# Recurrent attention and two expert layers on one core: the second batch's heads of a pair change places, and the start of the program is re-ordered

## The reference

```python
for t in range(S):                      # S = 768, per batch and head, D = 48
    y[t] = r[t] @ (state + (u * k[t]) outer v[t])
    state = w[t][:, None] * state + k[t] outer v[t]
...
x = y as 3072 rows of 384
h = x @ w_in                            # 384 -> 2048
x = (h * clip(h + 3, 0, 6) / 6) @ w_out # 2048 -> 384
xn = x / sqrt(mean(x * x) + 1e-6) * rms_g
x = (silu(xn @ w_gate) * (xn @ w_val)) @ w_out2   # 384 -> 1536 -> 384
```

## Time and profile before

| | us |
|---|---|
| median of 3 runs | 956.05 |
| lowest, highest | 953.65, 956.09 |
| the profiled execution's own time | 953.81 |
| its span | 952.1 |

### The profile page before, as it was taken

The page is one execution under the profiler, slowest core; times in us unless marked ns, Lnnn a source line. Parts: engine busy times, 40 slices in busy tenths (PEclk is TensorE's granted clock), DMA queues, the critical chain, the costliest instruction groups (busy, mean ns, idle before and its releaser), DMA issues.

```text
span 952.1 us, 17493 instructions
## 1 busy us (share of the span) xinstructions
PE 934.7 (98%) x7060; PEld 782.7 (82%) x7060; DVE 538.8 (57%) x781; ACT 358.1 (38%) x756; POOL 304.8 (32%) x246
## 2 busy tenths in 40 slices
PE   7899999999999999999999999999999999999998
PEld 7789988888888888888788888888888888888887
DVE  8897986667666676313784463463373373363332
ACT  4446544444444445435464123223223222313212
POOL 5687654455445454422561011011001101102000
PEclk9999999999999999999999999999999999999999
DMA  9855433223323222004222000010000001000000
GB/s 238 239 173 143 117 94 95 59 60 104 89 68 92 62 72 80 17 9 143 84 82 67 1 34 34 1 34 33 1 33 34 1 1 66 1 1 34 1 1 33
DMA packets 32927, 60.19 MB, mean 63 GB/s; under 512 B 6096, under 2 KB 19920, under 8 KB 32848
## 3 DMA queue, kind: packets, MB, share of 16 engines
q1 hardware_dynamic: 27392, 51.67, 18.9%
q10 hardware_dynamic: 5456, 7.41, 2.6%
HBM read 47.46 MB, written 9.44 MB: 60 GB/s over the span
## 4 chain that ended last, share of the span: by engine, by line
PE 88%; DVE 4%; ACT 3%; issue 2%; POOL 2%; DMA 1%; SPq 0%; ACTq 0%; DVEq 0%; POOLq 0%
PE acc L1051 32%; PE bank L1035 11%; PE bank L1037 11%; PE bank L1036 11%; PE pair L1036 5%; PE pair L1035 5%; PE pair L1037 5%; PE pair L1157 2%; DVE cum L682 1%; PE pair L1104 1%; PE acc L1247 1%; PE pair L1133 1%; PE bank L1125 1%; ACT att L501 1%; DVE ki L706 1%
## 5 line engine op out<-in xcount | busy, mean ns | idle before, releaser
L1051 PE MATMUL acc<-gs,w_dn 128*128 128x512 f32 (+1 forms) x1512 | 357.1, 382 | 0.7 <-POOL gs L928 0.7
L1051 PEld LDWEIGHTS acc<-gs,w_dn 128*128 128x128 f32 x1512 | 273.0, 188 | 55.0 <-POOL gs L928 0.9
L928 POOL TENSOR_TENSOR gs<-act_g,gs 128x512 fp32r<-128x512 f32 (+1 forms) x96 | 122.2, 1273 | 208.2 <-ACT gs L535 208.0
L1035 PE MATMUL bank<-xs,w_up 128*128 128x512 f32 (+1 forms) x480 | 180.1, 375 | 5.1 <-DMA xs<-y 1.4
L1037 PE MATMUL bank<-xs,w_up 128*128 128x512 f32 (+1 forms) x480 | 176.5, 368 | 0.0
L1036 PE MATMUL bank<-xs,w_up 128*128 128x512 f32 (+1 forms) x480 | 176.5, 368 | 0.0
L769 DVE SCALAR_TENSOR_TENSOR act_g<-act_u,bank 128x512 f32<-128x512 f32 (+1 forms) x112 | 68.0, 607 | 131.9 <-ACT act_u L527 131.0
L839 DVE TENSOR_TENSOR act_u<-act_u,bank 128x512 f32<-128x512 f32 x72 | 49.5, 687 | 149.2 <-ACT act_u L595 149.2
L527 ACT ACTIVATE act_u<-bank,half 128x512 f32<-128x512 f32 (+1 forms) x112 | 70.0, 625 | 137.9 <-PE bank L1037 137.8
L1035 PEld LDWEIGHTS bank<-xs,w_up 128*128 128x128 f32 x480 | 90.4, 188 | 23.2 <-DVE act_g L769 2.9
L599 ACT ACTIVATE gs<-act_g 128x512 fp32r<-128x512 f32 x72 | 45.5, 632 | 158.8 <-DVE act_g L845 158.8
(11 more groups left out here) (119 smaller groups left out, 1152.4 us busy)
## 6 DMA issues: line engine op xcount, KB each, us to landing
rkt<-in_rkT SPq DMA_DIRECT2D x48, 192.0 KB, 3.7
rkn<-in_rkN SPq DMA_DIRECT2D x22, 384.0 KB, 4.2
val<-in_valN SPq DMA_DIRECT2D x22, 256.0 KB, 3.0
dec<-in_decT SPq DMA_DIRECT2D x48, 97.5 KB, 2.7
x<-x_dram SPq DMA_DIRECT2D x6, 768.0 KB, 4.3
x_dram<-xo SPq DMA_DIRECT2D x5, 768.0 KB, 4.1
out<-xo SPq DMA_DIRECT2D x5, 768.0 KB, 3.2
raw_dn<-in_w_out SPq DMA_DIRECT2D x14, 192.0 KB, 4.5
```

Source lines behind the costliest of these rows:

```text
L928: pool.tensor_tensor(gs[:, f % GRING, 1, tok], act_g[:, f % 2, tok], gs[:, f % GRING, 0, tok].bitcast(F32), ALU.subtract).then_inc(s_glo, 1)
L1035: pe.matmul(dst, w_hi, x_hi, start=first, stop=False)
L1051: last = pe.matmul(ps_o[m][:, tok], w[:, wp, m * P:(m + 1) * P], gs[:, f % GRING, xp, tok], start=f == 0 and a == 0, stop=f == nf - 1 and ...
```

## The change

Three things.

1. In the second batch (b = 1) the two heads of a pair change places in everything that lies transposed or is summed per head (dec, rkt, and therefore cum, ki, rd, state, scores, att, bonus). Index i is now the place, and the head at it is i ^ b. The host lays out the inputs so; val and the outputs keep their order. `across` reads at the partitions of place i and writes at those of head i ^ b, so it uses all four quarters. It is no longer split: all 16 matmuls stand behind sums(g). bonuses(g) needs a u_h for each batch and so has 8 matmuls of 64 columns instead of 4 of 128, and u_b is loaded in two halves.
2. The start: SP issues only the four dec transfers and rms_s ahead of its wait; the four rkt transfers come from ACT's queue, ahead of u_h; val(0) and val(1) are issued behind u_h and ACT's first activation; ACT's wait for rkt(0) ahead of the weights is gone. `diag` and `mask` are made by ACT in four copies of 64 x 64 instead of by DVE in three instructions.
3. busy(24) becomes busy(18), busy(4) becomes busy(3).

```diff
-        NCONST = 4
+        NCONST = 5
...
                 for j in (1, 0):
-                    if g < 2 and j == 0:
-                        sp.wait_ge(zeroed[g], 1)
                     sp.dma_start(rkt[HI2 * j:HI2 * j + D, slot(g), :, :, :, :], rkT[g // SETS, g % SETS, j]).then_inc(ldR[slot(g)], 16)
...
             for g in range(2):
                 load_dec(g)
-                load_rk(g)
             sp.dma_start(rms_s[:, :], rms_g).then_inc(ldG, 16)
             landed(sp, ldR, 1, 2)
-            sp.dma_start(u_b[:, :], u.partition_broadcast(P)).then_inc(ldU, 16)
+            for b in range(PB):
+                sp.dma_start(u_b[T * b:T * (b + 1), :], u[b].partition_broadcast(T)).then_inc(ldU, 16)
...
             for g in range(2):
-                act.dma_start(val[:, g, :, :], valN[0, g]).then_inc(ldV[g], 16)
-            act.dma_start(u_h[0:DP, :, :], u_heads).then_inc(ldH, 16)
+                for j in (1, 0):
+                    if j == 0:
+                        act.wait_ge(zeroed[g], 1)
+                    act.dma_start(rkt[HI2 * j:HI2 * j + D, g, :, :, :, :], rkT[0, g, j]).then_inc(ldR[g], 16)
+            act.dma_start(u_h[0:DP, :, :, :], u_heads).then_inc(ldH, 16)
             act.wait_ge(s_half, 1)
             act.activation(y3[:, 0, 0:1], half[:, :], ACT.Copy)
-            landed(act, ldR, 0, 2)
+            for g in range(2):
+                act.dma_start(val[:, g, :, :], valN[0, g]).then_inc(ldV[g], 16)
+            for made, to, of in ((s_ident, diag, ident), (s_upper, mask, upper)):
+                act.wait_ge(made, 1)
+                for b in range(PB):
+                    rows = slice(T * b, T * (b + 1))
+                    act.activation(to[rows, :], of[rows, T * b:T * (b + 1)], ACT.Copy).then_inc(const, 1)
...
-            dve.wait_ge(s_ident, 1)
-            dve.tensor_tensor(diag[:, :], ident[:, 0:T], ident[:, T:P], ALU.add).then_inc(const, 1)
-            dve.wait_ge(s_upper, 1)
-            for b in range(PB):
-                rows = slice(T * b, T * (b + 1))
-                dve.tensor_copy(mask[rows, :], upper[rows, T * b:T * (b + 1)]).then_inc(const, 1)
...
-                                         val[T * b:T * (b + 1), q, 2 * p + j, 0:D], start=True, stop=True, skip_group_check=True)
+                                         val[T * b:T * (b + 1), q, 2 * p + (i ^ b), 0:D], start=True, stop=True, skip_group_check=True)
...
-                    last = pe.matmul(bonus_bank(g)[:, 2 * p:2 * p + 2], rk_t[g][0:DP, p, :], u_h[0:DP, p, :], start=True, stop=True)
+                    for b in range(PB):
+                        last = pe.matmul(bonus_bank(g)[T * b:T * (b + 1), 2 * p:2 * p + 2], rk_t[g][0:DP, p, T * b:T * (b + 1)],
+                                         u_h[0:DP, p, b, :], start=True, stop=True, skip_group_check=True)
...
-            def across(g, tiles):
-
+            def across(g):
+
+                pe.wait_ge(p_in, g + 1 - PLACED)
+                state_taken(pe, g - SETS)
                 for p in range(PAIRS):
-                    for j, b in tiles:
-                        rows = slice(HI2 * j, HI2 * j + D)
-                        last = pe.matmul(y_of(g)[rows, b, p * T:(p + 1) * T], state[rows, g % SETS, p, b, :],
+                    for i, b in TILES:
+                        rows = slice(HI2 * i, HI2 * i + D)
+                        heads = slice(HI2 * (i ^ b), HI2 * (i ^ b) + D)
+                        last = pe.matmul(y_of(g)[heads, b, p * T:(p + 1) * T], state[rows, g % SETS, p, b, :],
                                          rd[rows, slot(g), p, b, :], start=False, stop=True, skip_group_check=True)
-                return last
+                last.then_inc(p_y, 1)
...
                 last.then_inc(p_in, 1)
-                state_taken(pe, g - SETS)
-                across(g, TILES[0:2])
...
                 if g >= PLACED:
-                    pe.wait_ge(p_in, g + 1 - PLACED)
-                    across(g, TILES[2:4]).then_inc(p_y, 1)
+                    across(g)
...
-            busy(24)
+            busy(18)
...
-            busy(4)
+            busy(3)
```

More of the change, by code:

```diff
@@ L118, in build @@
         val3 = sa("val3", [P, PLACED, 2, KT, HI2])
-        u_h = sa("u_h", [P, PAIRS, 2])
+        u_h = sa("u_h", [P, PAIRS, PB, 2])
         last = sa("last", [P, LASTS, PAIRS * PB])
@@ L1005, in _ @@
                 split_up(f)
-            pool.wait_ge(ldU, 16)
+            pool.wait_ge(ldU, 16 * PB)
             rku_mul(2)
@@ L1101, in scores @@
                 for p in range(PAIRS):
-                    for j, b in TILES:
-                        rows = slice(HI2 * j, HI2 * j + D)
-                        last = pe.matmul(scores_of(g)[T * b:T * (b + 1), j, p * T:(p + 1) * T], ki[rows, q, p, b, :],
+                    for i, b in TILES:
+                        rows = slice(HI2 * i, HI2 * i + D)
+                        last = pe.matmul(scores_of(g)[T * b:T * (b + 1), i, p * T:(p + 1) * T], ki[rows, q, p, b, :],
                                          rd[rows, q, p, b, :], start=True, stop=True, skip_group_check=True)
@@ L1122, in sums @@
                 for p in range(PAIRS):
-                    for b, j in TILES:
-                        rows = slice(HI2 * j, min(HI2 * (j + 1), DP))
+                    for b, i in TILES:
+                        rows = slice(HI2 * i, min(HI2 * (i + 1), DP))
                         last = pe.matmul(sum_bank(g, b)[rows, p * D:(p + 1) * D], kiT[T * b:T * (b + 1), p, rows],
-                                         val[T * b:T * (b + 1), q, 2 * p + j, 0:D], start=True, stop=True, skip_group_check=True)
+                                         val[T * b:T * (b + 1), q, 2 * p + (i ^ b), 0:D], start=True, stop=True, skip_group_check=True)
                 last.then_inc(p_st, 1)
@@ L1133, in inside @@
                     last = pe.matmul(y_of(g)[HI2 * j:HI2 * (j + 1), b, p * T:(p + 1) * T], val[T * b:T * (b + 1), q, 2 * p + j, :],
-                                     att[T * b:T * (b + 1), q, j, p, :], start=p == 0, stop=False, skip_group_check=True)
+                                     att[T * b:T * (b + 1), q, j ^ b, p, :], start=p == 0, stop=False, skip_group_check=True)
                 return last
@@ L1140, in inside3 @@
                     last = pe.matmul(y_of(g)[HI2 * j:HI2 * (j + 1), b, k * T:(k + 1) * T], val3[T * b:T * (b + 1), g, j, k, :],
-                                     att[T * b:T * (b + 1), g, j, PAIRS - 1, :], start=False, stop=True, skip_group_check=True)
+                                     att[T * b:T * (b + 1), g, j ^ b, PAIRS - 1, :], start=False, stop=True, skip_group_check=True)
                 return last
@@ L1280, in chunks_transposed, with swapped, heads_of_u, chunks_swapped @@
     def chunks_transposed(x):
-        x = x.reshape(SETS, PB, PAIRS, 2, NT, T, D).transpose(4, 0, 3, 6, 2, 1, 5)
+        x = x.reshape(SETS, PB, PAIRS, 2, NT, T, D)
+        x = np.stack([x[:, 0], x[:, 1, :, ::-1]], axis=1).transpose(4, 0, 3, 6, 2, 1, 5)
         return np.ascontiguousarray(x)
+    def swapped(heads):
+        heads = heads.reshape(PAIRS, 2, D)
+        return np.stack([heads, heads[:, ::-1]])
+    def heads_of_u(u):
+        u = np.einsum("bpid,ij->idpbj", swapped(u), np.eye(2, dtype=np.float32))
+        u = np.pad(u, ((0, 0), (0, HI2 - D), (0, 0), (0, 0), (0, 0)))
+        return np.ascontiguousarray(u.reshape(P, PAIRS, PB, 2)[:DP])
+    def chunks_swapped(x):
+        x = x.reshape(SETS, PB, PAIRS, 2, NT, T, D)
+        x = np.stack([x[:, 0], x[:, 1, :, ::-1]], axis=1).transpose(4, 0, 1, 5, 2, 3, 6)
+        return np.ascontiguousarray(x).reshape(NT, SETS, C, DM)
     def chunks_natural(x):
@@ L1308 @@
         "valN": np.pad(chunks_natural(inputs["v"]), ((0, 0),) * 5 + ((0, HI2 - D),)).reshape(NT, SETS, C, H * HI2),
-        "rkN": np.stack([chunks_natural(inputs[n]).reshape(NT, SETS, C, DM) for n in "rk"], axis=3).reshape(NT, SETS, C, 2 * DM),
-        "u_heads": np.pad(np.einsum("pjd,ji->jdpi", inputs["u"].reshape(PAIRS, 2, D), np.eye(2, dtype=np.float32)),
-                          ((0, 0), (0, HI2 - D), (0, 0), (0, 0))).reshape(P, PAIRS, 2)[:DP],
-        "u": np.ascontiguousarray(inputs["u"]).reshape(DM),
+        "rkN": np.stack([chunks_swapped(inputs[n]) for n in "rk"], axis=3).reshape(NT, SETS, C, 2 * DM),
+        "u_heads": heads_of_u(inputs["u"]),
+        "u": np.ascontiguousarray(swapped(inputs["u"])).reshape(PB, DM),
         "w_in": into_slices(rows_of_x1(inputs["moe_w_in"])), "w_out": out_slices(inputs["moe_w_out"]),
```

3 lines of the change are left out of this document (2 added, 1 removed).

## The result

| | before | after |
|---|---|---|
| median (five executions each) | 954.69 | 948.20 |
| lowest, highest | 953.23, 956.09 | 946.26, 950.51 |
| profiled execution: own time, span | 953.81, 952.1 | 946.26, 944.5 |

The ratio is 0.9922, 95% interval 0.9904 to 0.9939: faster by 0.6 to 1.0%. The medians lie 6.5 us apart, the two profiled executions 7.55. The median of 956.05 from which the prediction counts was that of three executions; five have 954.69. Two executions took more than three times as long as the others, one of before (3300.02) and one of e12 (3310.72); they are counted in the medians and left out of the ratios.

The account below looks back on a forecast made before the run. PE was taken to bound from 130 to 420 us, and DVE work to hold it at the start; 6.2 + 0.4 + 0.9 + 2.0 = 9.5 off the median 956.05 gave 946.5 us, range 941 to 951.

Parts of the forecast that it names:

- across on four quarters: In each meet on PE, sums, across and drain take 1.00 us instead of 1.44, saving 0.44 (0.32 to 0.50).
- the part on the start: Earlier dec landing and an undisturbed second scan leave 2.0 us gained at 125 us (0.5 to 2.5).
- the sum of 6.2 + 0.4: Gain in PE's full stretch: 6.2 us from groups 8 to 21, 0.4 from groups 22 and 23.
- Groups 22 and 23: Meets without sums: across waits for inside's semaphore, yet each saves 0.2 us, both 0.4 (0 to 0.6).
- no overlap: Rival: in across, row halves sharing a bank go one after the other, nothing gained per meet; 954.0 us, 12%.
- one at a time: Rival: bank sharing makes each across matmul wait for the one before; slower, 968 us, 4%.
- landed at 4.4: At the start, dec(0) lands at 4.4 us, so the first scan on DVE gains 1.3 (0 to 1.4).
- The step on the second scan: Group 1's scan on DVE no longer stands behind POOL's multiply: 1.24 us instead of 2.30, 1.06 gained.
- PE's first up: PE's first up, at 22.56 us before, comes at most 2.3 earlier, near 20.3.
- the early meets: Groups 2 to 7 count only where the wait chain goes through PE, twice: 0.9 us (0 to 2.6).
- The start gives nothing: Rival: dec still lands at 5.6 us and rkt(1) late, so the start gains nothing; 948.5 us, 15%.

Follow-up runs that it names:

- e12: The kernel before with the new start alone, plus busy(8) and 15 unread filler matmuls in PE's start gaps; median 956.06 us, ratio 0.9996 to before.
- e8: The kernel after with another order of place and batch in across, so neighbours write the same bank from both row halves; 948.98 us.
- e5: The kernel after with ACT's first rkt transfer held until both dec(0) transfers have landed; median 949.65 us, ratio 0.994 to before.
- e1: The kernel after with the start and both busy counts as before, so the new layout and across only; median 947.85 us, ratio 0.9922 to before.
- e2: The kernel before with the new start alone, including busy(18) and busy(3); median 959.10 us, ratio 1.0032 to before.
- e4: The kernel before with all 16 across matmuls moved behind sums, still on two quarters; median 957.92 us, ratio 1.0033 to before.
- e6: The kernel after with diag and mask made by DVE again; 949.22 us.

## Why the prediction was right

The forecast was 946.5 in 941 to 951; 948.2 came out, faster. The gain is less well met than the time: 9.5 were forecast from a median of 956.05, and the medians of five lie 6.5 apart. Two thirds of the forecast (6.6 of 9.5) were right for their reason, across on four quarters; the part on the start was not, and that the time lies in the range all the same is owed to the range, which takes in a start that gives nothing. By its steps:

- **Across on four quarters.** Right in mechanism and size: 0.43 a meet against 0.44. Between pass 2 and pass 6 the sum of 6.2 + 0.4 came out as 5.82, 0.8 less. The period from one meet to the next, 226.47 - 207.04 = 19.43 before and 221.36 - 202.33 = 19.03 after, shrank by 0.40, so some 0.03 of each meet's 0.43 went back into the steps behind it. That is the part mis-sized: 14 x 0.40 = 5.6, and twice 0.13 for the groups below.
- **Groups 22 and 23.** From inside to the down, group 22 took 0.47 + 0.99 = 1.46 and takes 394.00 - 392.67 = 1.33: 0.13 gained for 0.2 forecast, with a gap of 0.26; group 23 gains 0.13 too (1.51 before, 1.38 after).
- **The banks.** The rivals "no overlap" (954.0) and "one at a time" (968) fell with the meet of 2.00 and with e8.
- **The start.** The step "landed at 4.4" failed: rkt's transfers moved beside dec, and it landed for a scan at 5.47 (e5: 3.84 with them held back). Of the 1.3 only 0.2 came. The step on the second scan was right (1.23 against 1.24 forecast, 1.07 gained), but I had overlooked ki(0) between them: from the end of the reciprocals to the second scan it is 11.38 - 10.13 = 1.25 instead of 11.05 - 10.34 = 0.71, since POOL's multiply of rkt(1), now from 9.65 to 10.91, has begun ahead of ki(0), which stands behind it and takes 1.22. (In before ki(0) began first, at 10.44 against 10.48, and took 0.69.) 0.20 + 1.07 - 0.54 = 0.73, so ki(1) began at 16.13, not 14.5. PE's first up came at 20.92, not 20.3. At pass 2 3.13 were gained against 2.9 forecast for start and early meets, but that they agree is luck: 1.05 of it goes with the clock of the two executions, the early meets gave 0.44 for 0.9, and the first up's 1.64, for 2.0, has the clock in it as well.
- **What that was worth.** In the one profiled execution the 2.0 seemed nearly right; in the medians it isn't there. e1, without the new start, has 947.85, and e2, with the new start alone, is 3 us slower than before. "The start gives nothing", 948.5, which had 15%, describes the median better than the forecast's sum does. What I had not named is PE's own instruction supply, and the clock beside it: the chain of waits of before shows neither, since in that execution the packet came at 16.76 and in time.
- **The sum.** In the profiled pair it closes: 3.13 + 5.82 - 1.40 = 7.55. The forecast of 9.5 was 1.95 too high there: 0.8 by groups 8 to 23, 1.4 by the reload of x, less 0.2 that stretches with unlike clocks gave more. It closes by number, not by cause.

Open are why the instruction packet comes late in some executions and whether the new start has to do with it, and why e2 is behind before, and e12 level with it, where the full change is not behind e1.

## What to carry to other kernels

When small matmuls use quarters of the array, look at which index sets the row half and which the column half: a host layout in which two indices cross (i ^ b) makes two quarters into four, and the starts of records, not their lengths, price it beforehand. A gain at a saturated start must be tested by itself and in several executions, since one profile can show a stretch at its best. And a stop of PE between two matmuls of one line, with no engine named, can be tested by counting instructions up to it in two kernels: the same count, and an instruction packet that starts shortly ahead of the end of the stop, mean that the instructions were late. And before a gain between two profiles is put down to a change, compare their granted clocks: one fall of 3.4 us was worth 1.6 us.

## What the runs showed of the hardware

- PE stood for 0.58 to 4.45 us in front of the same instruction by count in eight of fourteen profiled executions, and went on 2.5 to 2.9 us behind the start of the first 16 KB instruction packet (15.2 to 21.3 us).
- A fall of the granted clock to 0.50 for 3.4 us cost 1.6 us where PE was full (516.7 instead of 515.1 in e4 and e6), and 1.0 to 1.1 from 31.5 us (e6 and e8 against after).
- Two row halves wrote one bank on different partitions at full pace: 30 records and the drain in 0.56.
- The 16 narrower records of bonuses(0) start from 10.0 to 10.4, the 8 wide ones of before from 11.2 to 11.9: weight loads of 0.138 instead of 0.192 us.
- DVE's scan or ki and a POOL product of two operands in SBUF did not run side by side; the one that began later stood until the other ended. Scan behind POOL: 2.30 (before) and 2.21 (e5) instead of 1.23; ki(0) behind POOL: 1.22 (after) instead of 0.69; POOL behind DVE: 1.77 (before) and 2.19 (e5) instead of 1.27.
